# Second MLP of an attention and two-MLP kernel: nine of twelve blocks of gate and value by seven products of sums

## The reference

```python
# attention: q, k, v of shape (2, 8, 1152, 64)
q_pool = q.reshape(B, H, S // 2, 2, D).mean(axis=3)
scores = (1 / sqrt(D)) * q_pool @ k.T ; attn = softmax(scores) ; out = attn @ v
x = out.transpose(0, 2, 1, 3).reshape(1152, 512)
# first MLP, w_in 512 x 2048, w_out 2048 x 512
h = x @ w_in ; g = (a0 + a1*h + a2*h**2 + a3*h**3) / (1 + |b0|*|h| + |b1|*h**2 + 1e-6)
x = g @ w_out
# second MLP, w_gate and w_val 512 x 1536, w_out 1536 x 512
xn = x / sqrt(mean(x * x) + 1e-6) * rms_g
g = xn @ w_gate ; result = (g * sigmoid(g) * (xn @ w_val)) @ w_out
```

## Time and profile before

| | |
|---|---|
| median of three runs | 679.05 us (678.96 to 679.23) |
| span of the profiled execution | 677.1 us |
| TensorE busy | 667.8 us, 99% of the span |
| VectorE busy | 509.7 us, 75% |
| ScalarE busy | 430.9 us, 64% |
| GpSimd busy | 447.0 us, 66% |
| granted TensorE clock, mean | 1.000 |
| first products of both MLPs (L948), chain share, hb banks | 28% |
| second products (L1016), chain share | 20% |

### The profile page before, as it was taken

The page is one execution under the profiler, slowest core; times in us unless marked ns, Lnnn a source line. Parts: engine busy times, 40 slices in busy tenths (PEclk is TensorE's granted clock), DMA queues, the critical chain, the costliest instruction groups (busy, mean ns, idle before and its releaser), DMA issues.

```text
span 677.1 us, 12086 instructions
## 1 busy us (share of the span) xinstructions
PE 667.8 (99%) x3956; PEld 624.6 (92%) x3956; DVE 509.7 (75%) x1002; ACT 430.9 (64%) x1005; POOL 447.0 (66%) x452
## 2 busy tenths in 40 slices
PE   7899999999999999999999999999999999999998
PEld 5899999999999999998899999899999999999997
DVE  6899999999999958987889889967554444444433
ACT  5888989899898988988888888843511111111110
POOL 6887999999999979999989789760566540000000
PEclk9999999999999999999999999999999999999999
DMA  7657467665746320101110110111121210000012
GB/s 230 198 161 208 127 179 229 182 186 165 203 137 167 103 89 0 47 18 62 63 63 1 64 63 10 53 63 63 52 73 63 70 55 1 1 0 1 1 58 83
DMA packets 26157, 60.77 MB, mean 90 GB/s; under 512 B 3320, under 2 KB 8192, under 8 KB 25984
## 3 DMA queue, kind: packets, MB, share of 16 engines
q1 hardware_dynamic: 25824, 59.87, 29.1%
q10 hardware_dynamic: 288, 0.33, 0.2%
HBM read 43.78 MB, written 2.40 MB: 68 GB/s over the span
## 4 chain that ended last, share of the span: by engine, by line
PE 84%; POOL 11%; DMA 2%; issue 1%; DVE 1%; ACT 0%; SPq 0%; POOLq 0%; ACTq 0%; DVEq 0%
PE hb L948 28%; PE ob L1016 20%; PE sc L855 11%; PE sc L865 10%; PE pv_ps L883 6%; PE misc L883 5%; POOL num L806 3%; POOL num L808 3%; PE tb L948 2%; POOL wi_lo L719 1%; POOL wo_lo L719 1%; POOL wi_hi L717 1%; DMA wraw<-in_moe_w_out 1%; DMA qrawA<-in_q 1%; DMA wraw<-in_moe_w_in 1%
## 5 line engine op out<-in xcount | busy, mean ns | idle before, releaser
L1270 DVE TENSOR_REDUCE neg_part<-sc 128x1 f32<-128x384 f32 x216 | 106.8, 548 | 9.5 <-PE sc L855 8.0
L1279 DVE TENSOR_TENSOR pt_lo<-sc,pt_hi 128x384 fp32r<-128x384 f32 x216 | 107.5, 549 | 2.2 <-ACT pt_hi L1094 1.3
L1094 ACT ACTIVATE pt_hi<-sc 128x384 fp32r<-128x384 f32 x216 | 92.8, 494 | 24.8 <-PE sc L865 20.9
L1085 ACT ACTIVATE prob<-sc,neg_max 128x768 f32<-128x768 f32 (+1 forms) x144 | 106.2, 757 | 2.7 <-DVE neg_max L1272 2.7
L1016 PE MATMUL ob<-wo_hi,gt_hi 128*128 128x512 f32 x248 | 97.7, 394 | 1.3 <-DVE tok L1374 0.8
L1016 PE MATMUL ob<-wo_hi,gt_lo 128*128 128x512 f32 x248 | 97.3, 392 | 0.0
L1016 PE MATMUL ob<-wo_lo,gt_hi 128*128 128x512 f32 x248 | 96.5, 389 | 0.0
L948 PE MATMUL hb<-xt_hi,wi_hi 128*128 128x384 f32 x280 | 94.6, 338 | 0.0
L948 PE MATMUL hb<-xt_lo,wi_hi 128*128 128x384 f32 x280 | 94.1, 336 | 0.0
L948 PE MATMUL hb<-xt_hi,wi_lo 128*128 128x384 f32 x280 | 93.9, 335 | 0.0
L865 PE MATMUL sc<-ident,prob 128*128 128x128 f32 x648 | 82.4, 272 | 0.0
(11 more groups left out here) (184 smaller groups left out, 1732.3 us busy)
## 6 DMA issues: line engine op xcount, KB each, us to landing
wraw<-in_moe_w_out SPq DMA_DIRECT2D x6, 1024.0 KB, 5.0
krawB<-in_k SPq DMA_DIRECT2D x8, 576.0 KB, 4.3
qrawB<-in_q SPq DMA_DIRECT2D x8, 512.0 KB, 5.2
krawA<-in_k SPq DMA_DIRECT2D x7, 576.0 KB, 4.4
o_part<-o_sb SPq DMA_DIRECT2D x14, 288.0 KB, 3.7
qrawA<-in_q SPq DMA_DIRECT2D x7, 512.0 KB, 5.2
wraw<-in_moe_w_in SPq DMA_DIRECT2D x3, 1024.0 KB, 6.4
wraw<-in_moe_w_gate SPq DMA_DIRECT2D x3, 1024.0 KB, 5.1
```

The source lines that it names most:

```text
L1085: nc.scalar.activation(dst, sc[s][:, c0:c1, 0:KBANK], ACT.Exp, bias=neg_max[:, s:s + 1], accum_out=sum_parts[:, (s + i) % 2, i, part:part ...
L1094: nc.scalar.activation(pt[0][:, 3 * c:3 * c + 3, PT_COL[i]:PT_COL[i] + P], src, ACT.Copy).then_inc(pt_hi, 1)
L1270: nc.vector.tensor_reduce(neg_part[:, s, c:c + 1], sc[s][:, c, 0:KBANK], AX.X, ALU.max, negate=True).then_inc(part_done, 1)
L1279: nc.vector.tensor_tensor(pt[1][:, kt, col], src, pt[0][:, kt, col].bitcast(F32), ALU.subtract).then_inc(pt_lo, 1)
```

## The change

The weights of a block, gate and value with 512 rows, are seen as a matrix of 2 x 2 blocks: gate upper (`A11`), gate lower (`A12`), value upper, value lower (`A22`), of 256 rows and 128 features. The tokens are seen in halves: in each tile of 128 the first and the last 64 tokens, with 256 features above and below. In nine of the twelve blocks (f from 3) the eight block products are replaced by seven products of sums: S1 to S4 are sums of weights, T1 to T4 sums of tokens. Each block product is six matmuls (two k tiles by three terms) of 256 or 320 columns; part 0 holds half of the tiles 0 to 3, part 1 half of the tiles 4 to 8. A group is one block for one part, 42 matmuls. TensorE writes four banks (`hp`, a pair of banks, and `tb`); VectorE adds the products together and leaves gate and value of both halves in pairs of banks, on which the product with `rrow`, silu, the product and the split each run as one instruction over both banks.

The first three blocks stay eight plain products, in 12 units (block, part, half) of 24 matmuls of 256 or 320 columns. Behind them GpSimd forms the token sums out of copies of the turned tiles in SBUF (`turned`); the weights, not the tokens, are scaled by rms_g, in ScalarE (`scale_weights`). Raw weights come in 36 pieces of 256 KB into four places. 1/rms is applied to the result of the second product too (`accumulate2`). The turns of tokens and the tiles of the last chunk are reordered as shown.

In the shortened diff below removed lines are shown for the tables alone, and the lines are moved left by eight places.

```diff
-TURNS = [("x", 0), ("x", 1), ("x", 2), ("r", 0)] + [("x", t) for t in (3, 4, 5, 6)] + [("r", 1), ("x", 7), ("x", 8), ("r", 2)]
-RAW_AT = {45: 0, 46: 1, 47: 2}
+TURNS = [("x", 0), ("x", 1), ("x", 2), ("x", 3), ("r", 0), ("x", 4), ("x", 5), ("x", 6), ("x", 7), ("x", 8), ("r", 1), ("r", 2)]
...
+PLAIN = 3
+UNITS0 = [(f, part, half) for part in range(2) for f in range(PLAIN) for half in range(2)]
+GROUPS2 = [(f, part) for f in range(PLAIN, 12) for part in range(2)]
...
+SPLIT_ORDER = [("o", 0), ("o", 1), ("f", 3), ("o", 2), ("o", 3), ("f", 4), ("f", 5), ("f", 6), ("o", 4), ("o", 5), ("f", 7),
+       ("o", 6), ("o", 7), ("f", 8), ("f", 9), ("f", 10), ("o", 8), ("o", 9), ("f", 11), ("o", 10), ("o", 11)]
+F_FREE = 8
+SCALE_AT = {(3, 1): 5, (4, 0): 6, (5, 0): 7, (6, 1): 8, (7, 0): 9, (7, 1): 10, (9, 0): 11}
+EARLY_SCALE = {39: 0, 40: 0, 41: 0, 42: 0, 43: 1, 44: 1, 45: 1, 46: 1}
...
+    f, part = GROUPS2[g]
+    c, k = divmod(f, CHUNK)
+    if part == 1 and k == CHUNK - 1:
+        return [(c, t) for t in range(SPLIT if c < NC2 - 1 else TILES - 1)]
+    if part == 0 and k == 0 and c > 0:
+        return [(c - 1, t) for t in range(SPLIT, TILES)]
+    return []
...
+    def load_raw2(i):
+        kind, f = RAW2[i]
+        if i < RAWS:
+            sp.wait_ge(w_split, 8 * len(order))
+        elif RAW2[i - RAWS][0] == "o":
+            sp.wait_ge(o_split, 2 * RAW2[i - RAWS][1] + 2)
+        else:
+            g = RAW2[i - RAWS][1]
+            sp.wait_ge(f_split, f_base(g) + (4 if g < PLAIN else F_FREE))
...
+    def tokens_sums(t):
+        part, col = place(t)
+        x, full = turned[t % TURNED], xw_full[part]
+        odd = full[:, T1:].rearrange("p (a b) d n -> p b a d n", b=2)[:, 0]
+        pool.wait_ge(x_copied, t + 1)
+        nc.gpsimd.tensor_tensor(odd[:, :, :, col], x[:, :, HALF_TILE:P].rearrange("p (a d) n -> p a d n", a=2),
+                                x[:, 0:2].rearrange("p d (a n) -> p a d n", a=2), ALU.subtract).then_inc(t_full, 1)
+        pool.wait_ge(t_full, 3 * t + 1)
+        nc.gpsimd.tensor_tensor(full[:, T2, :, col], x[:, 2:4, HALF_TILE:P], full[:, T1, :, col], ALU.subtract).then_inc(t_full, 1)
+        pool.wait_ge(t_full, 3 * t + 2)
+        nc.gpsimd.tensor_tensor(full[:, T4, :, col], x[:, 2:4, 0:HALF_TILE], full[:, T2, :, col], ALU.subtract).then_inc(t_full, 1)
+    def tokens_sums_lo(t):
+        part, col = place(t)
+        pool.wait_ge(t_hi, t + 1)
+        y_hi, y_all, y_lo = (y[:, T1:].rearrange("p j d n -> p (j d) n")[:, :, col] for y in (xw[part][0], xw_full[part], xw[part][1]))
+        nc.gpsimd.tensor_tensor(y_lo, y_all, y_hi.bitcast(F32), ALU.subtract).then_inc(t_lo, 1)
...
+    def weights_last(f):
+        hi, lo, full, gate, value, n = weights(f)
+        nc.gpsimd.tensor_tensor(lo[:, A22], value[:, 2:4], hi[:, A22].bitcast(F32), ALU.subtract).then_inc(f_split, 1)
+        pool.wait_ge(f_split, n + 5)
+        nc.gpsimd.tensor_tensor(full[:, S4], gate[:, 2:4], full[:, S2], ALU.subtract).then_inc(f_split, 1)
+    def weights_hi(f):
+        hi, lo, full, gate, value, n = weights(f)
+        pool.wait_ge(f_split, n + 8)
+        nc.gpsimd.tensor_scalar(hi[:, S1:], full[:, S1:], 1.0, 0.0, ALU.mult, ALU.add).then_inc(f_split, 1)
+    def weights_lo(f):
+        hi, lo, full, gate, value, n = weights(f)
+        pool.wait_ge(f_split, n + 9)
+        nc.gpsimd.tensor_tensor(lo[:, S1:], full[:, S1:], hi[:, S1:].bitcast(F32), ALU.subtract).then_inc(f_split, 1)
...
+    plain_split(1)
+    tokens_sums(0)
+    tokens_sums(1)
     newton_root(0)
+    plain_split(2)
+    tokens_sums(2)
+    tokens_sums(3)
+    tokens_sums_lo(0)
+    tokens_sums_lo(1)
+    tokens_sums(4)
+    tokens_sums_lo(2)
+    tokens_sums(5)
+    tokens_sums_lo(3)
     newton_root(1)
+    for t in range(6, TILES):
+        tokens_sums(t)
+        tokens_sums_lo(t - 2)
+    tokens_sums_lo(TILES - 2)
+    tokens_sums_lo(TILES - 1)
...
+                pe.wait_ge(xb_lo, 3 * n + 3)
+                pe.wait_ge(x_copied, n + 1)
...
+    def group(g):
+        f, part = GROUPS2[g]
+        n, w, x = PART_COLS[part], slots[f % SLOTS], xw[part]
+        def block_product(bank, a, b, first, last):
+            for d in range(2):
+                for k, (i, j) in enumerate(((0, 0), (1, 0), (0, 1))):
+                    ins = nc.tensor.matmul(bank[:, 0:n], w[i][:, a, d], x[j][:, b, d], start=first and d == 0 and k == 0,
+                                           stop=last and d == 1 and k == 2, skip_group_check=True)
+            return ins
+        bank_a, bank_z = hp[g % 2][:, 0], hp[g % 2][:, 1]
+        if part == 0:
+            pe.wait_ge(f_split, f_base(f) + 10)
+        pe.wait_ge(t_lo, PART_TILES[part][1])
+        if g < 2:
+            pe.wait_ge(su_lo, len(UNITS0) - 1 + g)
         else:
+            pe.wait_ge(act_lo, g - 1)
+        block_product(bank_a, A11, B11, True, True).then_inc(p1_done, 1)
+        if g == 0:
+            pe.wait_ge(row_done, len(ROW_TILES))
+        else:
+            pe.wait_ge(val_low, g)
+        block_product(bank_x, S2, T2, True, True).then_inc(p6_done, 1)
+        block_product(bank_y, S3, T3, True, True).then_inc(p7_done, 1)
+        block_product(bank_z, S1, T1, True, True).then_inc(p5_done, 1)
+        pe.wait_ge(p1_copied, g + 1)
+        block_product(bank_a, A12, B21, False, True)
+        pe.wait_ge(u2_done, g + 1)
+        block_product(bank_x, A22, T4, True, True).then_inc(p4_done, 1)
+        pe.wait_ge(val_high, g + 1)
+        block_product(bank_z, S4, B22, False, True).then_inc(p3_done, 1)
...
+        for j, done in enumerate((su_gate, su_val)):
+            if m < 2:
+                pe.wait_ge(g_lo, UNITS * NC1 - 2 + 2 * m)
             else:
...
+    second_product(NC1 - 1, 3)
+    second_product(NC1 - 1, 4)
+    turn_tokens(2)
+    second_product(NC1 - 1, 5)
+    turn_tokens(3)
+    second_product(NC1 - 1, 6)
+    turn_scales(0)
+    second_product(NC1 - 1, 7)
+    turn_tokens(4)
+    second_product(NC1 - 1, 8)
+    turn_tokens(5)
+    for m in range(len(UNITS0)):
+        plain_unit(m)
+        if m < 3:
+            turn_tokens(6 + m)
+        if m == 4:
             turn_scales(1)
             turn_scales(2)
+    for g in range(len(GROUPS2)):
+        group(g)
+        for c, t in outs_behind(g):
+            second_product(NC1 + c, t)
...
+        if u in EARLY_SCALE:
+            f = EARLY_SCALE[u]
+            j = 2 * (u - 39 - 4 * f)
+            scale_weights(f, j, j + 2)
...
+    tokens_hi(0)
+    square(3)
+    g_hi_part(last - 1)
     root(0)
+    tokens_hi(1)
     g_hi_part(last)
+    scale_weights(2)
+    for t in range(2, 4):
+        tokens_copy(t)
+        square(t + 2)
+        tokens_hi(t)
     row_copy(0)
+    for t in range(4, 6):
+        square(t + 2)
+        tokens_copy(t)
+        tokens_hi(t)
+    square(8)
+    for t in range(3):
+        tokens_sums_hi(t)
+    for m in range(len(UNITS0)):
+        plain_silu(m)
+        if m < 3:
+            tokens_copy(6 + m)
+            tokens_hi(6 + m)
+        plain_hi(m)
+        if m < 6:
+            tokens_sums_hi(3 + m)
+        if m == 2:
+            root(1)
+        if m == 4:
             row_copy(1)
             row_copy(2)
+        if m == 6:
+            scale_weights(3)
+        if m == 10:
+            scale_weights(4)
+    for g in range(len(GROUPS2)):
+        first_copy(g)
+        if g > 0 and not outs_behind(g - 1):
+            silu(g - 1)
+            act_hi_part(g - 1)
+        if outs_behind(g):
+            silu(g)
+            act_hi_part(g)
+        if GROUPS2[g] in SCALE_AT:
+            scale_weights(SCALE_AT[GROUPS2[g]])
...
+    def second_sum(g):
+        n, u2 = PART_COLS[GROUPS2[g][1]], sums_p[g % 2]
+        dve.wait_ge(p6_done, g + 1)
+        dve.wait_ge(p1_copied, g + 1)
+        nc.vector.tensor_tensor(u2[:, 0:n], bank_x[:, 0:n], u2[:, 0:n], ALU.add).then_inc(u2_done, 1)
+    def value_high(g):
+        n, u2 = PART_COLS[GROUPS2[g][1]], sums_p[g % 2]
+        dve.wait_ge(p7_done, g + 1)
+        dve.wait_ge(u2_done, g + 1)
+        nc.vector.tensor_tensor(third_sum[:, 0:n], bank_y[:, 0:n], u2[:, 0:n], ALU.add).then_inc(u3_done, 1)
+        dve.wait_ge(p5_done, g + 1)
+        dve.wait_ge(u3_done, g + 1)
+        if g > 0:
+            dve.wait_ge(act_full, g)
+        nc.vector.tensor_tensor(val[:, 1, 0:n], hp[g % 2][:, 1, 0:n], third_sum[:, 0:n], ALU.add).then_inc(val_high, 1)
+    def sums_end(g):
+        part = GROUPS2[g][1]
+        n = PART_COLS[part]
+        z, both = hp[g % 2][:, 1, 0:n], hp[g % 2][:, :, 0:n].rearrange("p h (t n) -> p h t n", n=HALF_TILE)
+        dve.wait_ge(p4_done, g + 1)
+        nc.vector.tensor_tensor(val[:, 0, 0:n], bank_x[:, 0:n], third_sum[:, 0:n], ALU.add).then_inc(val_low, 1)
+        dve.wait_ge(p3_done, g + 1)
+        nc.vector.tensor_tensor(z, z, sums_p[g % 2][:, 0:n], ALU.add).then_inc(gate_sum, 1)
+        dve.wait_ge(gate_sum, g + 1)
```

(48 more changed lines are left out.)

544 lines of the change are left out of this document (348 added, 196 removed).

## The result

The changed kernel takes 683.32 us (median of four runs, 682.78 to 684.41) against 679.14 for the kernel before beside it: ratio 1.0061, 95% interval 1.0049 to 1.0073. A second measurement, on another chip (experiment 5), gave 684.68 and 1.0079 (1.0059 to 1.0099). The forecast was 676.5 us, faster than before, with a range up to 683; the kernel became slower, and 683.3 lies just outside that range.

The account below looks back on a forecast made before the run. In the second MLP only TensorE's own time was taken to count, until another engine makes it wait. Terms -12.8 + 0.5 + 7.1 + 0.7 + 1.5 + 0.5 = -2.5 took 679.05 to 676.5 us, range 670.5 to 683.

Parts of the forecast that it names:

- the hole's line: Before turn_tokens(2): VectorE and ScalarE wait for each other from activation1(46)'s end, 437.0, to tokens_lo(0)'s, 442.0.
- step 4: GpSimd's token sums, roots and block 3 sums up to the first group, ready at 495.9: TensorE waits 0.7 us.
- step 5: scale_weights(4), behind plain unit 10, waits for its DMA and delays group 0's first copy: a hole of 1.5 us (0 to 3).
- Step 1: Nine blocks by seven products: 11.09 us a block instead of 12.51, a gain of 12.8 us (12.0 to 13.6).
- Step 2: Three plain blocks: 96 matmuls a block instead of 72, 12.67 against 12.51 us, a loss of 0.5 us for three.
- the covered scalings in the groups: Scaling weights by g on ScalarE, 8 x 0.15 a block, hidden beside a group; uncovered it would cost 9 x 1.2.
- Step 3: Before turn_tokens(2): TensorE waits for token tile 0's bank until tokens_lo(0), a hole of 7.1 us (5 to 8.5).
- the clock falls in the hole: Rival, 25%: TensorE idle before turn_tokens(2) drops to 1.2 GHz, losing 3.5 or 1.8 us; 678.3 to 680, say 679.
- its shorter case: After the hole before turn_tokens(2), the clock stays low for half as long as the hole was: 1.8 us lost.
- GpSimd sets the pace: Rival, 20%: up to the first group GpSimd's instructions run slower than priced; 15% on top is 5.3 us, making 682.
- Step 6: Steady groups: TensorE's seventh product of 256-column groups behind 320-column ones fits by 0.2 us; 0.5 lost in all (0 to 3).

Follow-up runs that it names:

- experiment 4: Changed kernel with block 1's eight weight scalings moved from the first MLP's last units to behind g_hi_part(last), and plain_split(1) behind newton_root(0): 681.79 us, ratio 1.0040.
- experiments 2: Changed kernel with 36 matmuls of 512 columns that nobody reads put ahead of turn_tokens(2), to fill the first hole: 681.95 us, ratio 1.0042.
- Experiment 8: Changed kernel with root(1) ahead of the plain units and 36 unread matmuls of 512 columns in the first hole: 676.66 us, ratio 0.9953.
- experiment 15: Changed kernel with scale_weights(4) alone moved from behind plain unit 10 to the second group: 681.59 us, ratio 1.0037.
- experiment 11: Changed kernel with unread matmuls in both holes (36 before turn 2, 10 before turn_scales(1)) and nothing moved: 682.14 us, ratio 1.0045.
- Experiment 1: Changed kernel with root(1) called ahead of the plain units instead of behind plain unit 2: 678.38 us, ratio 0.9989.

## Why the prediction was wrong

The forecast had plain unit 0 at 455.1 and the span's end 2.8 us behind TensorE's 671.8, so 219.5 between them. Measured are 458.59 and 222.4. That is 3.5 us lost ahead of plain unit 0 and 2.9 behind it; with 0.35 more outside the span it is the 6.8 us missed. The 3.5 are the hole's line, 1.8 longer than forecast, and the clock's fall, 1.8, which the sum left out; the 2.9 are step 4's chain with step 5 at its end. Each of the three is under the 4.2 us by which the kernel became slower, so none alone turns "faster" into "slower".

- **Step 1 (nine blocks, -12.8): right.** A pair of groups takes 11.15 us (11.09 forecast).
- **Step 2 and the covered scalings in the groups: right.** Between 510 and 670 us TensorE has no wait. TensorE's own time behind plain unit 0 is 217.5 us, where the forecast without its waits has 216.8 (219.5 less 0.7, 1.5 and 0.5).
- **Step 3 (hole, +7.1): mechanism right, size off.** Turn 2 came at 443.77 (442.0 forecast) and waited for the bank. The line through VectorE and ScalarE took the 5.0 us forecast (438.7 to 443.7), but it began 1.7 late: VectorE ended `activation1(46)` at 438.7, not 437.0, because ScalarE was late. The scalings take 0.30 us each (eight in a row in 2.4, a pair 0.6), where I took 0.15; experiment 4 moved turn 2 by 1.6 when eight went.
- **The rival "the clock falls in the hole" came true** on top, as priced for its shorter case: 1.8 us. It was at 25% and should have been the forecast, since the step itself had TensorE idle for 7 us. The Trainium skill's rule ("TensorE: Matmul & The Clock Gate", "What's actually happening"), that the throttled state is the default and activity releases it, agrees with experiments 2 and 8, where work in the same hole kept the clock at 1.00.
- **Step 4 (GpSimd, +0.7): the step that failed.** Its instruction prices held: 1.29, 0.75, 2.41 us.

```profile
L1031 POOL TENSOR_TENSOR slot_lo<-slot_full,slot_hi 128x1024 fp32r<-128x1024 f32 x9 | 21.7, 2406 | 0.8
...
L990 POOL TENSOR_TENSOR x_lo<-x_full,x_hi 128x512 fp32r<-128x512 f32 x9 | 11.5, 1296 | 7.3 <-ACT x_hi L1545 7.3
```

  The error is in the term "wait for `root(1)` behind plain unit 2 and a table load of 1283 ns, to 469.3": two loads stand before `rinv` (472.25 and 473.76), and the chain has a third ahead of them, the first silu's (462.52). The forecast had GpSimd's root 14.2 us behind plain unit 0 (469.3 less 455.1); it came 16.85 behind it in all seven profiles with the late root, 2.6 more, the length of the two loads left out. The rival "GpSimd sets the pace" named 682 us and a chain on GpSimd up to the first group. The chain was there, but not for the reason given, since the instructions were no slower than forecast; that its time came close is luck.
- **Step 5 (+1.5): right in kind, too small.** The wait is 1.0 in this execution and up to 2.8 (2.6 and 0.2) where the second fall was missing; it is the tail of step 4's chain. Taking it away in experiment 15 shortened the stretch behind plain unit 0 by 2.4 to 3.1 us in the profiles, and the whole by 1.6 to 2.9 us by its ratio against the two of the changed kernel.
- **Step 6 (+0.5): right, nearer to nothing.** Behind the first group TensorE has no wait up to 670 us.

The forecast had no wait of TensorE at the plain units, and the second wait (474.2) refutes that. By the chain, taking away this wait alone would bring nothing, since GpSimd and the load end no earlier for it; that is argued, not shown, for only its fall was taken away (experiment 11).

Experiment 8, with the root early and the clock up, takes 676.66 us, close to the 676.5 forecast. That is in part luck: there the hole is longer than in the sum, and the sum's 0.7 and 1.5 for the first group are not there.

The Trainium skill, "ScalarE: Activation LUTs", section "Table sets: the hidden batching unit", has logarithm then exponential as one load, since one set holds both. Experiment 1's trace agrees where no silu ran before (463.39 and 463.61 above, no load between). The changed kernel's trace disagrees behind a silu: one load at 472.25 for the logarithm and another at 473.76 for the exponential.
